# Attention output transposed on two column halves of TensorE, and moved by DMA into the first GEMM's input

## The chip, the cores and the metric

One core of one Trainium2 chip runs the whole program. The metric is the device time of one execution in microseconds (us); the kernel before took 1053.1 us, the median of 3 runs (1052.9 to 1053.57).

## The reference

What is computed, cut to what matters. The mixer is a linear recurrence for each of 4 batches and 8 heads over 768 tokens, with a complex decay for each of the 48 key dimensions; then come two MLPs.

```
B, H, S, D = 4, 8, 768, 48
for t in range(S):                        # state S is complex, D x D for each batch and head
    new_re = ar * S_re - ai * S_im
    new_im = ar * S_im + ai * S_re
    S_re, S_im = new_re + k[t] (x) v[t], new_im
    y[t] = q[t] @ S_re
x = y.transpose(0, 2, 1, 3).reshape(3072, 384)
h = x @ w_in                              # 384 -> 2048
x = (h * clip(h + 3, 0, 6) / 6) @ w_out   # 2048 -> 384
out = (((x @ w1) * (x @ w2)) @ w3) @ w_out2
```

## The kernel before, in words

**Numbers.** Each large GEMM works on operands split into a high part (fp32r, rounded) and a low part (the remainder), in three products: high by high, high by low, low by high. Such a matmul is one record of the trace. Attention's own matmuls are plain fp32; one of these is two weight loads and two matmul records.

**Tiling.** Tokens come in 24 chunks of 128 (`NC`), three chunks make a unit of 384 tokens (`UNIT`), and there are 8 units (`NU`). A batch has 6 chunks, so that chunks 0, 6, 12 and 18 (`c == 0`) have no state from before them.

**The outer loop.** Every engine's program is written out by hand over `units` (from -2 to 7) and 16 slots `sl` in each. In slot `sl` of unit `u`, TensorE does one step of the first GEMM (`gemm1`, 9 matmuls of 384 columns into `hb`) and, two steps behind, one step of the second (`gemm2`, 9 matmuls into `acc`). Between them, in `u`'s slots, stand the pieces of attention of unit `u + 1`. For its chunk j (0, 1, 2) they are, by the table `STAGE`: decay sums `D` in slot 4j, transposes of Q and K (`TQ`, `TK`) in 4j+2 and 4j+3, scores `Sc` in 4j+4, output `Y` and state update `U` in 4j+5, and `turn_x` in 4j+6. So units -2 and -1 are a start without GEMM steps, and 21 of the 24 chunks (3 to 23) lie among the GEMM steps of units 0 to 6. The last part, after unit 7, is the second MLP; it has no attention in it.

**What a chunk's output does before.** `Y(g, i)` does four heads: for each head, `bQ[:, h*48:(h+1)*48]` is the sum of QbT as weights (96 rows, 128 columns) with the state `Z` moving (48 columns), if c > 0, and of the masked scores `AT` as weights (128 by 128) with `v_sb` moving (48 columns). `Y(g, 0)` stands behind `gemm1`, `Y(g, 1)` behind `gemm2`, and `U(g)` (8 matmuls with 96 weight columns and 48 moving ones into `bR`) behind that. The result has tokens on its partitions. ScalarE copies it to `xs` (`y_copied`), `turn_x` turns it with three 128x128 transposes into bank `bP`, ScalarE writes the high part `xH` and VectorE the low part `xL`, which the next unit's `gemm1` reads.

**Around it.** Banks: `bQ` and `bR` serve Q's and K's transposes, scores, output and state update in turn; `bP` serves decay sums, angle sums and `turn_x`. `TQ` of the next chunk is one slot behind `YU` and waits for `y_copied` and `state_out` (VectorE's last operation on `Z`, in `z_out`). VectorE does in a `YU` slot, in this order: the product `g_sb`, `rot` of the next chunk (`Qb`, then `Kb`, which waits for `U`), `z_out`, and a stage `pre` of the decays of the unit after next. All DMAs are on the one queue of SyncE, in the order of its program.

## Time and profile before

| what | value |
|---|---|
| median of 3 runs | 1053.1 us (1052.9 to 1053.57) |
| span of the profiled execution (first to last instruction) | 1051.8 us |
| so outside the span, against the median | 1.3 us |
| PE (TensorE matmul) busy | 1006.4 us, 96% of the span |
| PEld (weight loads, beside the matmuls) | 931.9 us, 89% |
| DVE (VectorE) | 528.6 us, 50% |
| ACT (ScalarE) | 428.5 us, 41% |
| POOL (GpSimd) | 366.7 us, 35% |

PE's busy time counts each matmul until its modelled end, and matmuls overlap; the distance from one record's start to the next one's is what a matmul costs in a full stream. A row of the timeline that merges several records gives the start of the first.

### The profile page before, as it was taken

To read this page: it belongs to the slowest core of one execution; us is meant where nothing else is said; L and a number is where in the kernel's file an instruction comes from. 1 tells how busy PE (TensorE), PEld (TensorE's weight loads), DVE (VectorE), ACT (ScalarE), POOL (GpSimd) and SP (SyncE) were. 2 spreads that over 40 slices of the span, in tenths; PEclk is the share of its full clock that TensorE was granted. 3 is DMA by queue.
4 is the path that set the end of the run, shared out by engine and by line. 5 is a ranking of instruction groups with operands and counts; after the bars stand their busy time and mean duration, and the time that the engine had idled before them with its cause. 6 is when DMAs were issued, how large, how long until landed. Compare 5 with 4: busy or idle time off the path is not lost.

```text
span 1051.8 us, 15149 instructions
## 1 busy us (share of the span) xinstructions
PE 1006.4 (96%) x5985; PEld 931.9 (89%) x5985; DVE 528.6 (50%) x669; ACT 428.5 (41%) x698; POOL 366.7 (35%) x294
## 2 busy tenths in 40 slices
PE   6887799999999999999999999999999999999996
PEld 3566699999999999999999999999888888888886
DVE  4678568668668758667857754334212121212111
ACT  4373454455454464454454452254312121212221
POOL 0261353453452452463363442135212221222111
PEclk9997699999999999999999999999999999999999
DMA  9252210110110021021020010060101010101000
GB/s 354 74 179 68 82 39 23 54 61 24 53 54 30 11 83 44 9 83 35 20 84 25 29 39 23 9 232 1 53 1 61 1 60 1 60 1 61 1 31 32
DMA packets 35176, 57.42 MB, mean 55 GB/s; under 512 B 2592, under 2 KB 29472, under 8 KB 35104
## 3 DMA queue, kind: packets, MB, share of 16 engines
q1 hardware_dynamic: 35104, 56.42, 16.1%
q8 instruction: 50, 0.82, 0.3%
q14 instruction: 22, 0.18, 0.1%
HBM read 45.40 MB, written 11.01 MB: 54 GB/s over the span
## 4 chain that ended last, share of the span: by engine, by line
PE 84%; issue 5%; DVE 4%; ACT 3%; POOL 2%; DMA 1%; SPq 0%; ACTq 0%; POOLq 0%; DVEq 0%
PE acc L712 16%; PE hb L692 14%; PE hb L913 10%; PE acc L935 7%; PE bQ L913 5%; PE bR L913 5%; PE bQ L792 4%; PE bQ L791 3%; PE bR L799 3%; PE bP L935 2%; PE bR L776 2%; PE acc L860 2%; PE bQ L776 2%; POOL gL L1312 2%; DVE W L1172 1%
## 5 line engine op out<-in xcount | busy, mean ns | idle before, releaser
L1312 POOL TENSOR_TENSOR gL<-g_sb,gH 128x384 fp32r<-128x384 f32 x128 | 159.6, 1247 | 272.1 <-ACT gH L1013 272.1
L1360 POOL TENSOR_TENSOR pL<-p_sb,pH 128x512 fp32r<-128x512 f32 x48 | 67.0, 1396 | 231.9 <-ACT pH L1099 231.9
L712 PE MATMUL acc<-gH,woutH 128*128 128x384 f32 x384 | 131.5, 342 | 3.8 <-ACT gH L1013 2.3
L1231 DVE SCALAR_TENSOR_TENSOR g_sb<-t_sb,hb 128x384 f32<-128x384 f32 x128 | 70.3, 549 | 127.4 <-ACT t_sb L1031 69.5
L712 PE MATMUL acc<-gH,woutL 128*128 128x384 f32 x384 | 128.8, 335 | 0.0
L712 PE MATMUL acc<-gL,woutH 128*128 128x384 f32 x384 | 128.6, 335 | 0.0
L1031 ACT ACTIVATE t_sb<-hb,cst 128x384 f32<-128x384 f32 x128 | 74.6, 583 | 86.6 <-PE hb L692 85.5
L1013 ACT CAST gH<-g_sb 128x384 fp32r<-128x384 f32 x128 | 65.5, 512 | 88.5 <-DVE g_sb L1231 88.5
L692 PE MATMUL hb<-xH,winH 128*128 128x384 f32 x384 | 95.4, 356 | 0.0
L692 PE MATMUL hb<-xL,winH 128*128 128x384 f32 x384 | 88.5, 338 | 0.0
L692 PE MATMUL hb<-xH,winL 128*128 128x384 f32 x384 | 87.7, 336 | 0.0
L712 PEld LDWEIGHTS acc<-gH,woutH 128*128 128x128 f32 x384 | 72.2, 188 | 7.9 <-ACT gH L1013 4.0
L1289 DVE TENSOR_TENSOR p_sb<-a_sb,bQ 128x512 f32<-128x512 f32 x24 | 16.5, 688 | 111.7 <-PE bQ L913 95.9
L712 PEld LDWEIGHTS acc<-gL,woutH 128*128 128x128 f32 x384 | 72.2, 188 | 0.0
L712 PEld LDWEIGHTS acc<-gH,woutL 128*128 128x128 f32 x384 | 72.1, 188 | 0.0
L792 PE MATMUL bQ<-v_sb,AT 128*128 128x48 f32 x384 | 71.7, 280 | 0.0
L1091 ACT COPY a_sb<-hb 128x512 f32<-128x512 f32 x48 | 28.2, 588 | 104.2 <-PE hb L913 104.2
L692 PEld LDWEIGHTS hb<-xL,winH 128*128 128x128 f32 x384 | 69.9, 190 | 0.0
L692 PEld LDWEIGHTS hb<-xH,winL 128*128 128x128 f32 x384 | 69.1, 189 | 0.0
L1289 DVE TENSOR_TENSOR p_sb<-a_sb,bR 128x512 f32<-128x512 f32 x24 | 16.5, 687 | 104.7 <-PE bR L913 99.7
L692 PEld LDWEIGHTS hb<-xH,winH 128*128 128x128 f32 x384 | 65.3, 191 | 0.4
L1099 ACT CAST pH<-p_sb 128x512 fp32r<-128x512 f32 x48 | 29.8, 621 | 85.4 <-DVE p_sb L1289 85.4
(166 smaller groups left out, 2214.0 us busy)
## 6 DMA issues: line engine op xcount, KB each, us to landing
AR<-in_a_re_dram SPq DMA_DIRECT2D x8, 576.0 KB, 4.1
AI<-in_a_im_dram SPq DMA_DIRECT2D x8, 576.0 KB, 5.2
q_sb<-in_q_dram SPq DMA_DIRECT2D x24, 192.0 KB, 2.5
k_sb<-in_k_dram SPq DMA_DIRECT2D x24, 192.0 KB, 3.0
v_sb<-in_v_dram SPq DMA_DIRECT2D x24, 192.0 KB, 2.4
x_dram<-x_sb SPq DMA_DIRECT2D x24, 192.0 KB, 2.7
out_dram<-o_sb SPq DMA_DIRECT2D x6, 768.0 KB, 4.3
w3t_sb<-in_moe_w_dram SPq DMA_DIRECT2D x8, 512.0 KB, 8.5
```

Of the source, the lines that this page charges most:

```text
L692: mm = pe.matmul(o, w[:, kk * DF1 + ft * P:kk * DF1 + (ft + 1) * P], xv(x, u)[:, kk, :], start=(i == 0), stop=(i == 8))
L712: mm = pe.matmul(acc[m][:, 0:UNIT], w[:, ft * DM + m * P:ft * DM + (m + 1) * P], gg[:, (n % 3) * UNIT:(n % 3 + 1) * UNIT], start=(ft == 0 ...
L776: mm = pe.matmul(bk[:, hh * P:(hh + 1) * P], heads(KbT, h, P)[0:D2, :], heads(QbT, h, P)[0:D2, :], start=True, stop=True)
L792: mm = pe.matmul(o, heads(AT, h, P), heads(v_sb[:, :], h, D), start=(c == 0), stop=True)
L913: mm = pe.matmul(bk[n % 2][:, :], w[:, kk * DF2 + ft * P:kk * DF2 + (ft + 1) * P], x[:, o:o + UNIT2], start=(i == 0), stop=(i == 8))
L935: mm = pe.matmul(acc2[tb][:, 0:DM], pp[:, o:o + P], w[:, ft * DM:(ft + 1) * DM], start=(ft == 0 and i == 0), stop=(ft == FT2 - 1 and i == 2))
L1013: act.copy(gH[:, (n % 3) * UNIT:(n % 3 + 1) * UNIT], g_sb[:, :]).then_inc(s["hswish_high"], 1)
L1031: act.activation(t_sb[:, :], hb[n % 2][:, 0:UNIT], ACT.Relu, bias=THREE_C).then_inc(s["relu_done"], 1)
L1231: dve.scalar_tensor_tensor(out=g_sb[:, :], in0=t_sb[:, :], scalar=6.0, in1=hb[n % 2][:, 0:UNIT], op0=ALU.min, op1=ALU.mult).then_inc(s["hs ...
L1289: dve.tensor_tensor(p_sb[:, (n % 2) * UNIT2:(n % 2 + 1) * UNIT2], a_sb[:, (n % 2) * UNIT2:(n % 2 + 1) * UNIT2], bb[n % 2][:, :], ALU.mult) ...
L1312: pool.tensor_tensor(gL[:, (n % 3) * UNIT:(n % 3 + 1) * UNIT], g_sb[:, :], gH[:, (n % 3) * UNIT:(n % 3 + 1) * UNIT].bitcast(F32), ALU.subt ...
L1360: pool.tensor_tensor(pL[:, (n % 3) * UNIT2:(n % 3 + 1) * UNIT2], p_sb[:, (n % 2) * UNIT2:(n % 2 + 1) * UNIT2], pH[:, (n % 3) * UNIT2:(n % ...
```

## The change

The output of a chunk is computed transposed. For each pair of heads, the state `Z` (96 rows) and `v_sb` (128 rows) are now the weights, 64 columns of each head (48 and 16 more, which belong to the next head or to a cleared pad), and QbT and AT are the moving operand, 128 columns. The even head's result goes to partitions 0 to 63 of `bQ`, the odd head's to 64 to 127. All heads of a chunk stand in one block behind `gemm2`. ScalarE rounds the bank to a high part and VectorE takes the low part, both into `yHL`; `turn_x`, `xs` and their waits are gone, and so are `xH` and `xL` as separate copies from `bP`. Six DMAs a chunk, from SBUF to SBUF, bring the 48 rows of each head to their place in `xHL`; the rows of `w_in` are laid out in the matching order outside the kernel (`w_in_x`).

```diff
-        xH = at("xH", 2 * KT * UNIT, F32R)
-        xL = at("xL", 2 * KT * UNIT, F32R)
+        xHL = at("xHL", 4 * KT * UNIT, F32R)
...
-        xs = at("xs", DM)
+        yHL = at("yHL", H * P, F32R)
...
+            def store_x(g):
+
+                u, j = divmod(g, CPU)
+                sp.wait_ge(s["y_low"], g + 1)
+                y = yHL[:, :].bitcast(F32).rearrange("p (b n) -> p b n", n=P)
+                x = xv(u).bitcast(F32)[:, :, j * P:(j + 1) * P]
+                done = s[f"x_dma{u % 2}"]
+                sp.dma_start(x[0:D, 0:6, :], y[0:D, 0:6, :]).then_inc(done, 16)
+                sp.dma_start(x[D:D2, 0:6, :], y[YM:YM + D, 0:6, :]).then_inc(done, 16)
+                sp.dma_start(x[D2:P, 0:2, :], y[0:P - D2, 6:8, :]).then_inc(done, 16)
+                sp.dma_start(x[D2:P, 2:4, :], y[YM:YM + P - D2, 6:8, :]).then_inc(done, 16)
+                sp.dma_start(x[D2:D2 + 16, 4:6, :], y[P - D2:D, 6:8, :]).then_inc(done, 16)
+                sp.dma_start(x[D2 + 16:P, 4:6, :], y[YM + P - D2:YM + D, 6:8, :]).then_inc(done, 16)
...
                 if ft == 0:
-                    pe.wait_ge(s["xT_high"], CPU * (u + 1))
-                    pe.wait_ge(s["xT_low"], CPU * (u + 1))
+                    pe.wait_ge(s[f"x_dma{u % 2}"], 16 * XD * CPU * (u // 2 + 1))
...
                 pe.wait_ge(s["q_turned"], g + 1)
                 if g > 0:
-                    pe.wait_ge(s["y_copied"], g)
+                    pe.wait_ge(s["y_high"], g)
+                    pe.wait_ge(s["y_low"], g)
                     pe.wait_ge(s["state_out"], g)
...
-                for h in range(4 * i, 4 * i + 4):
-                    o = bQ[:, h * D:(h + 1) * D]
+                for pair in (2 * i, 2 * i + 1):
+                    o = [bQ[YM * r:YM * (r + 1), pair * P:(pair + 1) * P] for r in range(2)]
                     if c > 0:
-                        pe.matmul(o, heads(QbT, h, P)[0:D2, :], heads(Z, h, D)[0:D2, :], start=True, stop=False)
-                    mm = pe.matmul(o, heads(AT, h, P), heads(v_sb[:, :], h, D), start=(c == 0), stop=True)
+                        for r in range(2):
+                            h = 2 * pair + r
+                            pe.matmul(o[r], Z[0:D2, h * D:h * D + YM], heads(QbT, h, P)[0:D2, :], start=True, stop=False)
+                    for r in range(2):
+                        h = 2 * pair + r
+                        mm = pe.matmul(o[r], v_sb[:, h * D:h * D + YM], heads(AT, h, P), start=(c == 0), stop=True)
...
-            def turn_x(g):
...
+                    if n is not None and n >= 2:
+                        gemm2(n - 2)
                     if (g := chunk(u, sl, "YU")) is not None:
                         Y(g, 0)
-                    if n is not None and n >= 2:
-                        gemm2(n - 2)
-                    if g is not None:
                         Y(g, 1)
                         U(g)
...
-                        act.copy(xs[:, :], bQ[:, 0:DM]).then_inc(s["y_copied"], 1)
...
+                            act.wait_ge(s["y_low"], g)
+                            act.wait_ge(s[f"x_dma{(g - 1) // CPU % 2}"], x_landed(g - 1))
+                        act.copy(yv(0), bQ[:, :].rearrange("p (i n) -> p i n", n=P)).then_inc(s["y_high"], 1)
...
                         z_out(g)
-                    if (g := chunk(u, sl, "X")) is not None:
...
+                        dve.wait_ge(s["y_high"], g + 1)
+                        dve.tensor_tensor(yv(1), bQ[:, :].rearrange("p (i n) -> p i n", n=P), yv(0).bitcast(F32),
+                                          ALU.subtract).then_inc(s["y_low"], 1)
```

TensorE's order at a chunk with state (slot 5 of a unit), before: the last matmuls of `gemm1` (L692), then the first half of `Y` (L791 with the state, L792 with the scores; four heads), then `gemm2` (L712).

```order
L692 MATMUL hb<-xH,winL 128x384 x3
L791 MATMUL bQ<-Z,QbT 128x48 [waits s_state_in,s_v_dma,s_scores_masked]
L792 MATMUL bQ<-v_sb,AT 128x48
L791 MATMUL bQ<-Z,QbT 128x48
L792 MATMUL bQ<-v_sb,AT 128x48
L791 MATMUL bQ<-Z,QbT 128x48
L792 MATMUL bQ<-v_sb,AT 128x48
L791 MATMUL bQ<-Z,QbT 128x48
L792 MATMUL bQ<-v_sb,AT 128x48
L712 MATMUL acc<-gH,woutH 128x384 [waits s_hswish_low,s_hswish_high]
L712 MATMUL acc<-gL,woutH 128x384
```

The same place after the change: `gemm2` (now L737) stands ahead, and behind its last matmul comes the output (L820 with the state, L823 with the scores), two heads in turn.

```order
L737 MATMUL acc<-gH,woutH 128x384
L737 MATMUL acc<-gL,woutH 128x384
L737 MATMUL acc<-gH,woutL 128x384
L820 MATMUL bQ<-QbT,Z 64x128 [waits s_state_in,s_v_dma,s_scores_masked]
L820 MATMUL bQ<-QbT,Z 64x128
L823 MATMUL bQ<-AT,v_sb 64x128 x2
L820 MATMUL bQ<-QbT,Z 64x128 x2
L823 MATMUL bQ<-AT,v_sb 64x128 x2
```

So the first half of `Y` moved behind `gemm2`, and each of the 16 matmuls now writes 64 partitions by 128 columns where it wrote 128 by 48. VectorE's order in the same slot and the next one, after the change; L1256 is the new subtraction.

```order
L1191 TENSOR_TENSOR Kb<-cs,GK 128x768 [waits s_kv_summed,s_k_decayed]
L1213 TENSOR_TENSOR Z<-bR,Z 96x384 [waits s_kv_summed]
L1215 TENSOR_TENSOR Z<-Z,Et 96x384 [waits s_state_added]
L1256 TENSOR_TENSOR yHL<-bQ,yHL 128x4x128 [waits s_y_high]
L1124 TENSOR_TENSOR W_65<-W_65,W_66 128x1152 [waits s_ln_mag_capped,s_exp_ln_mag]
L1230 SCALAR_TENSOR_TENSOR g_sb<-t_sb,hb 128x384 [waits s_hswish_low,s_relu_done]
L1203 TENSOR_TENSOR Z<-Z,Et 96x384 [waits s_state_out,s_half_decays_T]
L1240 COPY QbT<-bR 96x512 [waits s_qT_psum]
```

Before, the subtraction of the low part (`xL`, 384 columns) stood behind `QbT` in the next slot; it now stands ahead of `pre`'s W in the chunk's own slot. SyncE's order at the end of a unit (slots 13 to 15), after the change; the six DMAs are new, the others stood there before.

```order
L602 DMA v_sb<-in_v_dram 128x384 [waits s_kv_summed]
L639 DMA xHL<-yHL 48x6x128 [waits s_y_low]
L640 DMA xHL<-yHL 48x6x128
L641 DMA xHL<-yHL 32x2x128
L642 DMA xHL<-yHL 32x2x128
L643 DMA xHL<-yHL 16x2x128
L644 DMA xHL<-yHL 16x2x128
L589 DMA AR<-in_a_re_dram 128x3x384 [waits s_turns_low,s_angles_summed]
L589 DMA AI<-in_a_im_dram 128x3x384
```

The six stand behind the load of the next chunk's V and ahead of the loads of a unit's decays.

## Rows read from the trace of the kernel before

**Rows 1.** The page, section 1: busy us (share of the span) xinstructions, by engine.

```profile
PE 1006.4 (96%) x5985; PEld 931.9 (89%) x5985; DVE 528.6 (50%) x669; ACT 428.5 (41%) x698; POOL 366.7 (35%) x294
```

**Rows 2.** Windows: stretch, length, busy by engine (xcount), PEclk, DMA share, GB/s.

```profile
0.00:98.00 98.00, 75.53 (x338) 51.54 (x338) 67.01 (x69) 50.59 (x62) 27.80 (x18) 0.94 0.50 173
98.00:127.00 29.00, 22.43 (x82) 19.47 (x83) 17.46 (x21) 9.35 (x14) 7.47 (x5) 0.56 0.33 102
455.40:537.30 81.90, 81.16 (x559) 79.75 (x559) 58.66 (x76) 41.07 (x72) 36.31 (x32) 1.00 0.14 44
```

**Rows 3.** PE's waits over the whole span: us in total, times, longest.

```profile
PE acc L712 <- ACT gH L1013: 2.3, 6, 0.4
PE bP L847 <- DVE xL L1259: 1.4, 1, 1.4
```

**Rows 4.** Timeline of PE in a chunk's slot: start, us, line, out<-in, xcount.

```profile
468.88 0.35 PE L791 MATMUL bQ<-Z,QbT 96*128 96x48 f32 x2
...
470.62 0.42 PE L712 MATMUL acc<-gH,woutH 128*128 128x384 f32 x1
...
470.88 0.34 PE L712 MATMUL acc<-gL,woutH 128*128 128x384 f32 x1
...
472.29 0.32 PE L791 MATMUL bQ<-Z,QbT 96*128 96x48 f32 x2
...
474.01 1.52 PE L799 MATMUL bR<-v_sb,Kb 128*96 128x48 f32 x16
...
475.36 0.78 PE L692 MATMUL hb<-xH,winH 128*128 128x384 f32 x3
```

**Rows 5.** Timeline of PE at `turn_x`, alone in its slot.

```profile
442.55 0.49 PE L818 MATMUL bP<-cst,xs 128*128 128x128 f32 x3
442.80 0.78 PE L692 MATMUL hb<-xH,winH 128*128 128x384 f32 x3
```

**Rows 6.** Timeline of PE at `TQ`: four transposes with 96 weight columns each.

```profile
457.13 0.60 PE L759 MATMUL bQ<-cst,Qb 128*96 128x128 f32 x4
457.57 0.60 PE L759 MATMUL bR<-cst,Qb 128*96 128x128 f32 x4
```

**Rows 7.** Timeline of PE at `halves_sums`: six matmuls with 32 weight columns, between others.

```profile
575.76 1.52 PE L799 MATMUL bR<-v_sb,Kb 128*96 128x48 f32 x16
577.11 0.35 PE L726 MATMUL bP<-logrH,cstR 128*32 128x384 f32 x1
...
578.17 0.68 PE L692 MATMUL hb<-xH,winH 128*128 128x384 f32 x3
```

**Rows 8.** Timeline of DVE and PE between a chunk's `U` and the next `TQ`.

```profile
475.64 0.96 DVE L1192 TENSOR_TENSOR Kb<-cs,GK 128x768 f32<-128x768 f32 x1 [2.02 <-PE bR L799]
...
477.10 0.79 DVE L1216 TENSOR_TENSOR Z<-Z,Et 96x384 f32<-96x384 f32 x1
...
478.59 0.60 PE L759 MATMUL bQ<-cst,Qb 128*96 128x128 f32 x4
```

**Rows 9.** Timeline from a unit's last `U` to the next unit's first `gemm1`.

```profile
520.51 0.42 PE L844 MATMUL bP<-TH,cstR 128*128 128x384 f32 x1
...
521.31 0.56 DVE L1216 TENSOR_TENSOR Z<-Z,Et 96x384 f32<-96x384 f32 x1
...
528.62 0.70 PE L692 MATMUL hb<-xH,winH 128*128 128x384 f32 x3
```

**Rows 10.** The DMA queue's packets, MB, share; one issue; one load's time to landing.

```profile
q1 hardware_dynamic: 35104, 56.42, 16.1%
...
476.41 0.43 SPq L587 DMA_DIRECT2D k_sb<-in_k_dram  x1
...
v_sb<-in_v_dram SPq DMA_DIRECT2D x24, 192.0 KB, 2.4
```

**Rows 11.** Timeline of PE at chunk 2 of the start, output and state update.

```profile
101.15 0.49 PE L791 MATMUL bQ<-Z,QbT 96*128 96x48 f32 x2
...
107.85 2.76 PE L799 MATMUL bR<-v_sb,Kb 128*96 128x48 f32 x16
```

More of the change, by code:

```diff
@@ L141, in mixer_mlp_kernel @@
         MID = cstR[:, 2 * P:3 * P]
-        HALF = [cstR[:, 3 * P + 32 * j:3 * P + 32 * (j + 1)] for j in range(CPU)]
+        HALF = [cstR[:, 3 * P + 2 * (CPU - 1 - j):3 * P + 2 * (CPU - 1 - j) + 32] for j in range(CPU)]
         w3t_sb = at("w3t_sb", FT2 * DF2, F32, wout_at)
@@ L258, in heads, with xv, x_landed, yv @@
             return t[:, h * w:(h + 1) * w]
-        def xv(t, u):
-            n = KT * UNIT
-            return t[:, (u % 2) * n:(u % 2 + 1) * n].rearrange("p (k n) -> p k n", k=KT)
+        def xv(u):
+            n = 2 * KT * UNIT
+            return xHL[:, (u % 2) * n:(u % 2 + 1) * n].rearrange("p (b n) -> p b n", n=UNIT)
+        def x_landed(g):
+            u, j = divmod(g, CPU)
+            return 16 * XD * (CPU * (u // 2) + j + 1)
+        def yv(part):
+            return yHL[:, :].rearrange("p (i c n) -> p i c n", c=2, n=P)[:, :, part, :]
         units = range(-2, NU)
@@ L642, in _ @@
                         load_v(g + 1)
+                    if (g := chunk(u, sl, "X")) is not None:
+                        store_x(g)
                     if sl == 15 and u + 3 < NU:
@@ L649, in _ @@
                     if u == NU - 2 and sl == 15:
-                        sp.wait_ge(s["xT_low"], NC)
-                        sp.wait_ge(s["xT_high"], NC)
+                        for i in range(2):
+                            sp.wait_ge(s[f"x_dma{i}"], 16 * XD * CPU * NU // 2)
                         sp.wait_ge(s["kv_summed"], NC)
@@ L689, in gemm1 @@
                 i = 0
-                for w, x in ((winH, xH), (winH, xL), (winL, xH)):
+                for w, part in ((winH, 0), (winH, 1), (winL, 0)):
                     for kk in range(KT):
-                        mm = pe.matmul(o, w[:, kk * DF1 + ft * P:kk * DF1 + (ft + 1) * P], xv(x, u)[:, kk, :],
+                        mm = pe.matmul(o, w[:, kk * DF1 + ft * P:kk * DF1 + (ft + 1) * P], xv(u)[:, 2 * kk + part, :],
                                        start=(i == 0), stop=(i == 8))
@@ L800, in U @@
                 mm.then_inc(s["kv_summed"], 1)
-            def turn_x(g):
-                a, j = divmod(g, CPU)
-                pe.wait_ge(s["y_copied"], g + 1)
-                if j == 1 and a + 1 < NU:
-                    pe.wait_ge(s["half_decays"], a + 2)
-                elif j < 2:
-                    pe.wait_ge(s["decays"], g + 2)
-                elif a == 0:
-                    pe.wait_ge(s["sin_turns"], CPU + 1)
-                elif a + 1 < NU:
-                    pe.wait_ge(s["sin_turns"], CPU * (a + 1) + 2)
-                else:
-                    pe.wait_ge(s["xT_low"], g)
-                for kk in range(KT):
-                    mm = pe.transpose(bP[:, kk * P:(kk + 1) * P], xs[:, kk * P:(kk + 1) * P], IDENT)
-                mm.then_inc(s["xT_psum"], 1)
             def angle_sums(p, j):
@@ L880, in _ @@
                     a, p = u + 1, u + 2
-                    for stage, do in (("D", decay_sums), ("TQ", TQ), ("TK", TK), ("S", Sc), ("X", turn_x)):
+                    for stage, do in (("D", decay_sums), ("TQ", TQ), ("TK", TK), ("S", Sc)):
                         g = chunk(u, sl, stage)
@@ L1305, in _ @@
             EARLY_LOW = (0, 12, 13)
+            for t in (v_sb, Z):
+                pool.memset(t[:, DM:DM + YM - D], 0.0).then_inc(s["pads_cleared"], 1)
             def low_g(n):
@@ L1371, in constants, with x_rows @@
     m = ((mid < src) & (src <= dst)).astype(np.float32) - ((dst < src) & (src <= mid)).astype(np.float32)
-    half = np.zeros((P, CPU, 32), np.float32)
-    for j in range(CPU):
-        half[:, j, 2 * j], half[:, j, 2 * j + 1] = i <= mid, i > mid
+    half = np.zeros((P, 32 + 2 * (CPU - 1)), np.float32)
+    half[:, 2 * (CPU - 1)], half[:, 2 * CPU - 1] = i <= mid, i > mid
     return np.concatenate([np.eye(P, dtype=np.float32), np.full((P, 1), 1.0, np.float32), np.full((P, 1), 3.0, np.float32),
-                           tri, np.ones((P, P), np.float32), m, half.reshape(P, CPU * 32)], 1)
+                           tri, np.ones((P, P), np.float32), m, half], 1)
+def x_rows():
+    rows = []
+    for kk, (h, e) in enumerate(((H - 2, 0), (H - 1, 0), (None, P - D2))):
+        rows += range(2 * kk * D, (2 * kk + 2) * D)
+        rows += (range(h * D, h * D + P - D2) if h is not None else
+                 [*range((H - 2) * D + e, (H - 1) * D), *range((H - 1) * D + e, H * D)])
+    return np.array(rows)
 def kernel(**inputs):
```

65 lines of the change are left out of this document (25 added, 40 removed).

## The prediction

> **What bounds the kernel now.** I read the page first, for who is busy: PE 96% of the span, the next engine (DVE) 50% [rows 1]. A mean over stages can mislead, so next the windows: over one whole unit (81.9 us, from one unit's slot 1 to the next one's) PE is busy for 81.16, DVE for 58.66, and the granted clock is 1.00, the 2.4 GHz level [rows 2]. PE's own waits come third: among the GEMM steps they are small, 2.3 us in six times for the largest [rows 3]. So in units 0 to 6 time is what TensorE's stream costs, and the timeline tells what a piece of it costs by the distance between starts, since records overlap.
>
> **The prices in the stream.** In a chunk with state, the output's first half takes 468.88 to 470.62, 1.74 us, and the second 472.29 to 474.01, 1.72 us: 3.46 us for 16 matmuls, that is 32 records of 108 ns [rows 4]. The state update has 16 records in 474.01 to 475.36, 1.35 us or 84 ns each [rows 4]. Both move only 48 columns; they differ in weight columns, 128 against 96. So weights set the pace, at 24 ns for 32 columns, and 64 columns would be 60 ns by the same line. A four-transpose group with 96 weight columns, which by weights would take 84 ns each, takes 0.44 us, 110 ns each [rows 6]: there the 128 moving columns set it. A transpose is one pass as one record of an fp32 matmul is, so I take 110 ns as the price of 128 moving columns.
>
> **The change, part by part.** Per matmul record it swaps 128 weight columns and 48 moving ones for 64 and 128.
>
> 1. *Output.* If the two halves of the array work at the same time, two records share 110 ns of moving, 55 each, and their weights take 60 each: weights set it, 32 x 60 = 1.92 us in place of 3.46. If not, a record is 110 ns and the output 3.52 us. No row of before has two column halves at work, so both ends stay for the range. The order written, even head, odd head, even, odd, lets a half's second record run beside the other's first, and weight loads already run beside matmuls in this trace (PEld 931.9 us beside PE 1006.4 [rows 1]). I take the first end, nearer to what these loads do: 1.54 us less a chunk, 0.77 where c = 0. Among GEMM steps there are 18 chunks with state and three without: 18 x 1.54 + 3 x 0.77 = 30.0 us.
>
> 2. *One block.* Each return from plain fp32 to a GEMM step costs 0.26 us to the second start (470.62 to 470.88) [rows 4] where 0.18 is the pace of these matmuls (six in 1.06 us [rows 7]): 0.08 us. One return a chunk goes: 21 x 0.08 = 1.7 us.
>
> 3. *turn_x.* 442.55 to 442.80, 0.25 us [rows 5], and 0.08 more where it stands alone, which is one of three: 0.28 on the mean, 21 x 0.28 = 5.9 us.
>
> 4. *Turning the array into halves and back*, 42 times. Nothing in before shows it for certain. The nearest row is the sum with 32 weight columns: it starts 1.35 us behind the state update's start, as long as that update takes anyway, and six of them with the return take 1.06 us, 0.18 each [rows 7]. That is zero, if those 32 columns run as a part of the array. The other end is a stream that has to run empty: a record's length over its pace, 0.34 less 0.18, up to the whole 0.34 [rows 4]. I take 0.16 x 42 = 6.7 us lost, between 0 and 14.
>
> The Trainium skill ("TensorEngine Tiling (Array Packing)", Key Properties) says that a change of tiling mode drains TensorE. By it the term is not zero; what a drain costs it doesn't say. The same skill ("TensorE: Matmul & The Clock Gate", Part 3, Measured speedup vs the span model) gives 2.38 times for three column tiles, 0.79 of ideal; for two at that rate, an estimate, a record would cost 69 ns, the output 2.21 us, and the whole 5.7 us less gain than mine. No run here shows it yet.
>
> 5. *New waits on bQ.* The next TQ now waits for the low part, behind ScalarE's rounding and VectorE's queue. At j = 0, counted from the end of U at 475.36 [rows 4]: Kb from 475.64, Z's last product ends at 477.89, and the subtraction over 512 columns adds about 0.75 (0.56 for 384 [rows 9], by columns): 478.64, where TQ starts at 478.59 [rows 8]. All of this hangs from U's end and moves with it, so TQ is some 0.2 us late with its semaphore, 7 x 0.2 = 1.4 us. At j = 1 halves_sums stands between, 1.06 us [rows 7], and covers it; at j = 2 the next TQ is five slots on. Behind the subtraction on VectorE are pre and the next g_sb, 0.75 later; the old subtraction behind QbT is gone, so the queue is only 0.2 longer a chunk, some 59 of 77.5 us. On ScalarE two operations become one. Without this cover each 0.1 us costs 0.7.
>
> 6. *The DMAs.* 8 blocks of 96 rows are 768 packets of 512 bytes a chunk. SyncE issues one in 0.43 us and a load of 192 KB lands in 2.4 [rows 10]. Chunks j = 0 and 1 have slots to spare. The last has not: from U's end (520.51) the low part is there at 521.87 + 0.75, so +2.1; six issues of 0.43 end at +4.7; the last lands 2.4 from its start, +6.7. The next unit's first gemm1 stood at +8.1 [rows 9], less turn_x 0.34: +7.8. Other bound: 35104 packets in 16.1% of 16 engines' span are 77 ns each [rows 10], 48 an engine are 3.7 us, all added to the first landing: 2.1 + 2.4 + 3.7 = +8.2. So between 1.1 us early and 0.4 late; at the last boundary, where no angle sums stand between (8 matmuls of 0.18), 1.4 less. I take 1.6 us in all, 0 to 5. Queued behind them on SyncE are the loads of decays, a unit ahead of their use, and V's load three slots on: nothing urgent.
>
> 7. *The start.* Chunks 0 to 2 lie before the GEMMs. Chunk 2's output takes 101.15 to 107.85, 6.70 us [rows 11], as the clock there is 0.56, near the 1.2 GHz level [rows 2]. At twice 60 ns a record it would be 3.84, 2.9 less; chunk 1 gives 1.5, chunk 0 0.8, the transposes 1.4 and the wait of an angle sum for xL 1.4 [rows 3]: 8.0 if all of it is on the path. But PE is busy only 75.53 of the first 98 us [rows 2], and weight splitting runs beside. I take half, 4.0, between 0 and 8.
>
> Sum: 30.0 + 1.7 + 5.9 - 6.7 - 1.4 - 1.6 + 4.0 = 31.9 us off the profiled span of 1051.8, so 1019.9; with the 1.3 us outside it, 1021 us against the median of 1053.1.
>
> **The rivals.** 0.2% of this time, 2.1 us, is about what a measurement can tell from no change.
>
> - *Halves overlap in part*, a record at 85 ns, midway: output 2.72 us, 0.74 less a chunk: 19.5 x 0.74 = 14.4 in place of 30.0, and a us less at the start: 1038 us. Two moving operands at a time is what no row shows.
> - *No overlap*, 110 ns: the output loses 19.5 x 0.06 = 1.2, parts 2 and 3 gain 7.6, parts 4 to 6 cost 9.7, the start gives 2: 1054 us, no change. For it: every record in the trace works alone on the array, and starts are in order.
> - *Slower: weights of a half aren't loaded ahead.* Then a record is 60 + 110 = 170 ns, the output 5.44 us, 19.5 x 1.98 = 38.6 lost, in place of 30.0 gained, and nothing at the start: 1094 us. It decides from 108 ns a record: there the output costs what it did, and the other terms cancel (7.6 - 9.7 + 2). Against it: PEld and PE are both busy 80 of 82 us in a unit [rows 2], so loads do run ahead, if with the whole array.
> - *The DMAs are late at each unit's end*, by 3 us rather than 0.2, if packets of this kind are much slower than 77 ns: 8 x 3 = 24 us, 1043 us. The packets of before speak against it [rows 10].
>
> The Trainium skill ("TensorE: Matmul & The Clock Gate", Part 3, The mechanism) has a rule for the slower one: weight loads overlap matmuls only when the row groups differ. Here both halves use all rows. The trace of before contradicts it for the whole array, since all its matmuls use the same rows [rows 2]; for halves no row shows it.
>
> **How the numbers follow.** Full overlap 0.60 (its own range 1011 to 1031, from parts 4 to 7's bounds); part overlap 0.15; none 0.11; weights in series 0.07; late DMAs 0.07. The likeliest is 1021. The range 1011 to 1048 takes in the first two and the late DMAs, and leaves out the other two. Faster: 0.60 + 0.15 + 0.06 of the late DMAs = 0.81; same, most of no overlap: 0.07; slower 0.12.
>
> **What would show it.** The new output's 32 records between gemm2's last start and U's first: near 1.9 us for my case, 3.5 for none, 5.4 for series. Even and odd head's records should lie on each other. The starts around the block, less pace, give part 4. TQ at slot 6 with a wait for yHL gives part 5, the first gemm1 of a unit with a wait for a DMA part 6. A unit should take about 77.5 us for 81.9. I am wrong if records stand 110 ns or more apart, or if gemm1 waits over 1 us at every unit.

## The result and the profile after

The changed kernel takes 1009.59 us, the median of 4 runs (1009.13 to 1010.04), against 1053.0 for the kernel before in the same session (1052.54 to 1053.57): ratio 0.9589, 95% interval 0.9578 to 0.96. That is 43 us less; the prediction said 1021, range 1011 to 1048. The mechanism was the one forecast, its size was not: the profiled span went from 1051.8 to 1007.3, 44.5 less, where 31.9 was worked out. The profiled execution of the changed kernel is its fastest, 1009.13, with 1.8 us outside the span, and in all other runs it is 1.7 to 2.0; by that measure the one of the kernel before is its slowest, 1053.57, and the 1.3 that the prediction took outside its span is 0.5 too small. So 1.1 us of the 44.5 is not in the medians.

The page of the changed kernel, busy times and the DMA queue (packets, MB, share of 16 engines), beside [rows 1, 10]:

```profile
PE 960.0 (95%) x5913; PEld 877.4 (87%) x5913; DVE 528.4 (52%) x669; ACT 422.3 (42%) x674; POOL 364.9 (36%) x296
...
q1 hardware_dynamic: 55840, 65.84, 20.5%
...
xHL<-yHL SPq DMA_DIRECT2D x48, 144.0 KB, 2.6
```

PE is still the bound, and 46 us of its busy time are gone. The largest of the new transfers land in 2.6 us (median).

Windows of the changed kernel: two whole units, then the three stretches of [rows 2] (the second stretch of [rows 2] had a granted clock of 0.56):

```profile
349.20:501.60 152.40, 150.89 (x1088) 145.72 (x1086) 114.98 (x150) 80.69 (x135) 71.66 (x63) 1.00 0.21 63
0.00:98.00 98.00, 73.77 (x338) 48.48 (x340) 67.38 (x72) 49.79 (x60) 28.30 (x20) 0.96 0.53 181
98.00:127.00 29.00, 21.27 (x123) 19.35 (x124) 23.69 (x25) 14.17 (x22) 17.94 (x12) 0.78 0.43 130
127.00:662.00 535.00, 529.55 (x3813) 511.72 (x3812) 371.07 (x488) 270.04 (x453) 232.03 (x206) 1.00 0.22 67
```

Two units take 152.4 us in place of 162.6, so the mean unit takes 76.2 in place of 81.3 (the 81.9 of [rows 2] is the longer unit of a pair). The granted clock is 1.00, the 2.4 GHz level, in both kernels among the GEMM steps from 127 us on; between 98 and 127 us it is 0.78 after the change.

The new block in the timeline of PE, in a chunk with state. The last `gemm2` matmul stands at 440.62, then come the output (L820 from the state, L823 from the scores), `U` (L830), and the return to `gemm1` (L717); 447.21 and 447.59 are the last `gemm2` matmul before the next `TQ`, and that `TQ`:

```profile
440.62 0.34 PE L737 MATMUL acc<-gH,woutL 128*128 128x384 f32 x1
440.88 0.44 PE L820 MATMUL bQ<-QbT,Z 96*64 96x128 f32 x4
441.15 0.39 PE L823 MATMUL bQ<-AT,v_sb 128*64 128x128 f32 x4
...
442.48 0.39 PE L823 MATMUL bQ<-AT,v_sb 128*64 128x128 f32 x4
442.79 1.56 PE L830 MATMUL bR<-v_sb,Kb 128*96 128x48 f32 x16
444.18 1.29 PE L717 MATMUL hb<-xHL,winH 128*128 128x384 f32 x6
...
447.21 0.34 PE L737 MATMUL acc<-gH,woutL 128*128 128x384 f32 x1
447.59 0.61 PE L784 MATMUL bQ<-cst,Qb 128*96 128x128 f32 x4
```

How to read it: the output's 32 records begin at 440.88 and `U` follows at 442.79, 1.91 us in place of 3.46 [rows 4]. Groups of four records start 0.22 us apart (441.15 to 442.48 is six groups in 1.33), 55 ns a record, half of the 110 ns that 128 moving columns cost in a transpose [rows 6]. A change of mode, from the whole array to halves or back, shows as the excess over the pace: 440.62 to 440.88 is 0.26 for 0.17, so 0.09 going in, and the last group takes 0.31 for 0.22, 0.09 coming out. `TQ` starts 0.38 behind the last matmul, 0.2 over the pace.

PE's waits after the change (us in total, times, longest):

```profile
PE hb L717 <- DMA xHL<-yHL: 3.9, 2, 3.3
...
PE bP L851 <- issue: 1.9, 4, 0.9
```

The new DMAs are waited for twice: 3.3 us ahead of the very first `gemm1`, and 0.6 ahead of the last unit. At the ordinary unit's end nothing is waited for: in the one from 482 us on, the state update ends at 485.78, the last of the six DMAs is issued at 491.03 and lands in some 1.9 us, and `gemm1` of the next unit starts at 493.52.

**Where the 44.5 us came from.** VectorE's evacuation of `acc` marks the end of each unit: in the kernel before at 211.5 (unit 0) and 694.1 (unit 6), after at 196.7 and 650.5. The first `gemm1` starts at 118.39 before and 110.19 after. So 8.2 us come ahead of the first `gemm1`, 6.6 more in unit 0, 28.8 in the six units after it, and 0.9 behind them, in a stretch that the change doesn't touch and that takes 356.5 to 357.7 us in all the profiles of this study. The prediction, split in the same way: 4.0, 4.0 (a seventh of its 27.9 among GEMM steps), 23.9 and 0.

Units come in pairs of different length; "two units" below is the time between the ends of units 1 and 3, which was 162.6 in the kernel before (292.2 to 454.8) and is 152.4 in the changed one (272.7 to 425.1).

### The profile page after: what moved, and what is told of

It is laid out like the page before. It is cut to its first block, busy times and chain, and to the rows that moved or that the text cites. A ratio compares the mean times of both kernels' runs of the same rounds, so it can differ in the third digit from the quotient of the medians.

```text
span 1007.3 us, 15116 instructions
## 1 busy us (share of the span) xinstructions
PE 960.0 (95%) x5913; PEld 877.4 (87%) x5913; DVE 528.4 (52%) x669; ACT 422.3 (42%) x674; POOL 364.9 (36%) x296
## 2 busy tenths in 40 slices
DMA packets 55913, 66.84 MB, mean 66 GB/s; under 512 B 4896, under 2 KB 50208, under 8 KB 55840
## 3 DMA queue, kind: packets, MB, share of 16 engines
q1 hardware_dynamic: 55840, 65.84, 20.5%
## 4 chain that ended last, share of the span: by engine, by line
PE 80%; issue 7%; DVE 5%; ACT 3%; POOL 3%; DMA 1%; SPq 1%; ACTq 0%; POOLq 0%; DVEq 0%
PE acc L737 15%; PE hb L717 14%; PE hb L916 10%; PE acc L938 8%; PE bR L916 5%; PE bQ L916 5%; PE bR L830 3%; POOL gL L1310 3%; PE bP L938 2%; PE bR L801 2%; PE acc L864 2%; PE bQ L801 2%; PE bQ L823 2%; PE bQ L820 2%; PE bQ L784 1%
## 5 line engine op out<-in xcount | busy, mean ns | idle before, releaser
L1310 POOL TENSOR_TENSOR gL<-g_sb,gH 128x384 fp32r<-128x384 f32 x128 | 155.4, 1214 | 253.5 <-ACT gH L1016 209.5
L717 PE MATMUL hb<-xHL,winH 128*128 128x384 f32 x768 | 162.8, 347 | 3.9 <-DMA xHL<-yHL 3.9
L717 PEld LDWEIGHTS hb<-xHL,winH 128*128 128x128 f32 x768 | 133.6, 191 | 5.0 <-DMA xHL<-yHL 4.6
L737 PE MATMUL acc<-gH,woutH 128*128 128x384 f32 x384 | 129.1, 336 | 4.1 <-ACT gH L1016 2.6
L737 PE MATMUL acc<-gH,woutL 128*128 128x384 f32 x384 | 128.6, 335 | 0.0
L737 PE MATMUL acc<-gL,woutH 128*128 128x384 f32 x384 | 128.3, 334 | 0.0
L717 PE MATMUL hb<-xHL,winL 128*128 128x384 f32 x384 | 87.7, 336 | 0.0
L737 PEld LDWEIGHTS acc<-gH,woutH 128*128 128x128 f32 x384 | 72.1, 188 | 6.9 <-ACT gH L1016 4.3
L737 PEld LDWEIGHTS acc<-gL,woutH 128*128 128x128 f32 x384 | 72.1, 188 | 0.0
L737 PEld LDWEIGHTS acc<-gH,woutL 128*128 128x128 f32 x384 | 72.1, 188 | 0.0
L717 PEld LDWEIGHTS hb<-xHL,winL 128*128 128x128 f32 x384 | 69.3, 189 | 0.0
L1323 POOL TENSOR_TENSOR GQ<-GQ,q_sb 128x384 f32<-128x384 f32 x24 | 24.3, 1011 | 82.2 <-ACT GK L1008 78.5
L938 PE MATMUL acc<-woH,pL 128*128 128x384 f32 x144 | 48.7, 338 | 0.0
L938 PE MATMUL acc<-woH,pH 128*128 128x384 f32 x144 | 48.6, 338 | 0.0
```

Of the source, the lines that this page charges most:

```text
L717: mm = pe.matmul(o, w[:, kk * DF1 + ft * P:kk * DF1 + (ft + 1) * P], xv(u)[:, 2 * kk + part, :], start=(i == 0), stop=(i == 8))
L737: mm = pe.matmul(acc[m][:, 0:UNIT], w[:, ft * DM + m * P:ft * DM + (m + 1) * P], gg[:, (n % 3) * UNIT:(n % 3 + 1) * UNIT], start=(ft == 0 ...
L938: mm = pe.matmul(acc2[tb][:, 0:DM], pp[:, o:o + P], w[:, ft * DM:(ft + 1) * DM], start=(ft == 0 and i == 0), stop=(ft == FT2 - 1 and i == 2))
L1310: pool.tensor_tensor(gL[:, (n % 3) * UNIT:(n % 3 + 1) * UNIT], g_sb[:, :], gH[:, (n % 3) * UNIT:(n % 3 + 1) * UNIT].bitcast(F32), ALU.subt ...
```

## The experiments

Each was timed in five rounds or more against the kernel before, whose median in these sessions was 1052.3 (experiments 1, 3, 4 and 9), 1052.7 (5, 7, 8 and 10) and 1053.2 (2, 6 and 11). An interval behind a ratio is the 95% interval. "Two units" and "unit 0" are read from the one profiled execution of each kernel. The start varies by itself: the kernel before and experiment 5 have the same program ahead of the first GEMM step and the same order of the two engines in experiment 8, and chunk 2's output begins at 101.15 us in one and at 99.95 in the other. So a difference of a us or so at the start tells nothing.

**1. The two halves: even heads, then odd heads, within each four.**

```diff
-                for pair in (2 * i, 2 * i + 1):
-                    ... (both heads of a pair in turn)
+                for r in range(2):
+                    for pair in (2 * i, 2 * i + 1):
+                        ... (one head at a time, two of a half in a row)
```

> The changed kernel with another order inside the output block: four even-head matmuls on the lower column half, then four odd-head ones on the upper, instead of even and odd alternating. Same matmuls, same number. If the gain of the output comes from both halves working at once, this order undoes most of it: records 110 ns apart except at the changes of half, some 3.3 us a block for 1.8, so 1.5 us for each of 18 chunks, 0.7 for each of 3, and the start: about 1040 us. If the halves need not overlap and the smaller weights alone made it cheaper, it stays at 1010.

1021.45 us (1020.25 to 1022.67), ratio 0.9702 (0.9689 to 0.9715). Neither end. Timeline of PE in this kernel, the whole output block (L820 from the state, L821 from the scores):

```profile
448.73 0.43 PE L820 MATMUL bQ<-QbT,Z 96*64 96x128 f32 x2
449.00 0.38 PE L821 MATMUL bQ<-AT,v_sb 128*64 128x128 f32 x2
449.22 0.44 PE L820 MATMUL bQ<-QbT,Z 96*64 96x128 f32 x4
449.44 0.44 PE L821 MATMUL bQ<-AT,v_sb 128*64 128x128 f32 x4
...
450.93 0.38 PE L821 MATMUL bQ<-AT,v_sb 128*64 128x128 f32 x2
451.24 1.56 PE L828 MATMUL bR<-v_sb,Kb 128*96 128x48 f32 x16
```

In the program the first eight records are all one half's. In the trace only the first four stand alone (448.73 and 449.00, two records in 0.22, so 110 ns each); from 449.22 groups of four start 0.22 to 0.28 apart, nearly as many as two halves at work give. The odd half's first matmul began four records ahead of its turn. The block takes 2.51 us, 0.60 more than 1.91, and two units take 155.5 (277.5 to 433.0), 3.1 more. Of the six chunks in two units one is the first of its batch (`c == 0`) and has half the output, so 5.5 x 0.60 = 3.3 is what the rows give.

**2. All even heads of the chunk, then all odd ones** (the wait for the masked scores of all eight heads now stands ahead of both).

```diff
-                for pair in (2 * i, 2 * i + 1):
+                for pair in range(4):
+                    r = i
```

> The changed kernel with all even heads (one column half) of a chunk's output first, 16 records, and then all odd heads, 16 records. With four even and four odd records in turn the halves still ran beside each other, one some four records behind. Theory A, TensorE looks ahead over a few instructions only, so that halves 16 records apart can't lie on each other except at the seam: most of the 32 records then cost 110 ns, the output some 3.3 to 3.5 us in place of 1.9, 19.5 x 1.5 = 29 us and 2 or 3 at the start, 1040 us; and as PE then stays 4.6 us in plain fp32 matmuls a chunk, the clock may fall in mid-kernel as it did with one long block of the old output, which would make it longer still. Rival B, it looks as far ahead as its queue goes: as with halves in turn, 1021 us or less.

1036.84 us (1035.92 to 1041.12), ratio 0.9852 (0.9834 to 0.9871). Theory A holds: the output goes back to 3.28 us. Timeline of PE in this kernel:

```profile
424.96 0.43 PE L820 MATMUL bQ<-QbT,Z 96*64 96x128 f32 x2
425.23 0.38 PE L821 MATMUL bQ<-AT,v_sb 128*64 128x128 f32 x2
...
426.33 0.44 PE L820 MATMUL bQ<-QbT,Z 96*64 96x128 f32 x4
426.55 0.44 PE L821 MATMUL bQ<-AT,v_sb 128*64 128x128 f32 x4
426.82 0.38 PE L820 MATMUL bQ<-QbT,Z 96*64 96x128 f32 x2
...
428.24 1.56 PE L828 MATMUL bR<-v_sb,Kb 128*96 128x48 f32 x16
```

Two records in 0.22 nearly everywhere, 110 ns each; only at the seam (426.33 to 426.82) do eight records share 0.49 us, the last four of one half and the first four of the other. TensorE ran some four records ahead of the order, no more, in both kernels. Two units take 159.7 (285.7 to 445.4), 7.3 more than in the changed kernel, for 5.5 x 1.37 = 7.5 by the rows, and the window of that stretch shows the clock at 1.00. This is nearly the whole worth of the overlap: 19.5 x 1.37 = 27 us, with all else of the change in place.

**3. 48 weight columns rather than 64** (`v_sb[:, h * D:(h + 1) * D]` and the same of `Z`).

> The changed kernel with 48 weight columns for each head instead of 64, so without the 16 that belong to the next head; the rows they filled in the bank are not used by anything. In the changed kernel a record takes 55 ns. If the 128 moving columns of two records at a time set that (110 halved), nothing changes: 1009.6, same. If the 64 weight columns set it, as the prediction had it, a record goes to about 45 ns at most and the time falls by 0.3 us a chunk, 6 us: 1004.

1011.31 us (1008.93 to 1013.07), ratio 0.9602 (0.9588 to 0.9617). The interval overlaps that of the changed kernel, and two units take 152.4 (276.2 to 428.6), as in the changed kernel. So the 128 moving columns set the 55 ns, and a line from weight columns had nothing to say here. The profiled run was later at its start alone (end of unit 0 at 200.3 for 196.7), of which experiment 8 tells more.

**4. The output in two blocks again, around `gemm2`.**

```diff
-                    if n is not None and n >= 2:
-                        gemm2(n - 2)
                     if (g := chunk(u, sl, "YU")) is not None:
                         Y(g, 0)
+                    if n is not None and n >= 2:
+                        gemm2(n - 2)
+                    if g is not None:
                         Y(g, 1)
```

> The changed kernel with the first half of the output put back ahead of the second GEMM's step, as before the change; the second half stays behind it. It adds two changes between whole array and halves for each of 21 chunks and nothing else. The trace of the changed kernel shows about 0.09 us extra at the way in and 0.14 to 0.2 at the way out. If that is the price: 21 x 0.25 = 5 us, 1015 us. If a change costs nothing: 1010. If it drains for a record's whole length each way: 21 x 0.7 = 15 us, 1024.

1019.03 us (1017.63 to 1019.64), ratio 0.9681 (0.9667 to 0.9694). Two units take 154.4 (276.3 to 430.7), 2.0 more, or 0.33 a chunk for a second pair of changes and one return, 7 us over 21 chunks. Predicted were 0.32 and 0.08; the expectation of 0.25 a chunk, 1015 us, was too low, and a drain of a whole record each way, 1024, too high. The profile's end of unit 0 is 2.5 us later (199.2), of which experiment 8 tells more.

**5. The one block alone: the kernel before, with its old output in one block behind `gemm2`** (the same edit, the other way round).

> The kernel before with one part of the change alone: all eight heads of a chunk's output behind the second GEMM's step. It takes away one return from plain fp32 to a GEMM step a chunk, 21 x 0.08 = 1.7 us: 1051.3. If the first half ahead of that step had hidden a wait for the second GEMM's operands, it loses as much or more: 1053 to 1056.

1070.12 us (1067.37 to 1074.24), ratio 1.0169 (1.0148 to 1.019). A miss of both: 17 us slower, not 2 faster. Windows of 2 us in this kernel (PE busy, the others, then the granted clock, DMA share, GB/s); the output stands at 309.28 to 312.78 and `U` at 312.78 to 315.05:

```profile
310.00:312.00 2.00, 2.00 (x21) 2.00 (x20) 1.04 (x3) 0.20 (x1) 0.96 (x1) 1.00 0.00 0
312.00:314.00 2.00, 2.00 (x19) 2.00 (x18) 0.49 (x1) 1.02 (x2) 0.00 (x0) 0.77 0.00 0
314.00:316.00 2.00, 2.00 (x11) 2.00 (x11) 0.63 (x1) 1.01 (x2) 0.91 (x1) 0.50 0.00 0
...
320.00:322.00 2.00, 2.00 (x17) 1.95 (x16) 0.60 (x2) 0.69 (x2) 0.00 (x0) 1.00 0.00 0
```

PE is busy 2.00 of 2.00 us throughout, and the clock falls to the 1.2 GHz level at 313.1, 0.3 us into the state update, and stays there until 319.9: for 6.8 us, 4.8 of them GEMM steps. What PE did before it fell: 3.8 us of plain fp32 matmuls that move 48 columns each, the output and the first records of `U` in one piece. In the kernel before, a `gemm2` stood between the halves of that piece. This happens in some chunks, not all: its units take 82.0, 88.1, 80.6, 86.4, 80.6 and 79.8 us, where those of the kernel before take 80.7, 81.9, 80.7, 81.9, 80.6 and 76.8.

**6. Each output matmul twice, in the changed kernel** (`for pair in (2 * i, 2 * i + 1) * 2`; the second time into the same place).

> The changed kernel with each output matmul of a chunk issued twice (the second time into the same place, from the start again; the output is the same). It adds 32 records at the pace of the new form and no change of mode. Theory A, what lets the clock fall in the one long block of the old form is matmuls that move few columns, not the length of the plain fp32 stretch: the new form moves 128 columns in two halves, the granted clock stays at the 2.4 GHz level in units 0 to 6, and the kernel takes 19.5 x 1.76 = 34 us more, and 2 to 5 at the start: 1046 us. Rival B, the length of the stretch away from the GEMM steps decides (now some 5 us a chunk, as in the one long block of before): the clock falls in some chunks and the time is 1055 us or more.

1049.58 us (1046.65 to 1051.12), ratio 0.9966 (0.9956 to 0.9977). Theory A holds. Two units take 162.1 (288.6 to 450.7), 9.7 more. By 1.76 us (32 x 55 ns) it should be 5.5 x 1.76 = 9.7. Windows of 100 us in this kernel:

```profile
200.00:300.00 100.00, 99.00 (x735) 95.84 (x734) 69.86 (x89) 49.80 (x86) 49.70 (x41) 1.00 0.22 70
...
400.00:500.00 100.00, 99.24 (x810) 95.59 (x809) 73.69 (x92) 48.17 (x79) 40.77 (x36) 1.00 0.20 58
```

Output and `U` together now take 5.1 us a chunk (3.7 and 1.4), longer than the 3.8 after which the clock fell in experiment 5, in plain fp32 as there, and the clock doesn't move. It doesn't in experiment 2 either (3.28 and 1.4), where the halves work one at a time. So the length of the stretch away from the GEMM steps doesn't explain the fall. What differs from experiment 5 is the form of the output, 128 moving and 64 weight columns a record in place of 48 and 128; no run changes one of the two alone. The 3.5 us beyond the expectation are at the start: in this profile the first `gemm1` stands 7.5 us later than in the changed kernel (117.66 for 110.19) and the end of unit 0 11.5, with the slow order of experiment 8.

**7. `turn_x` twice, in the kernel before** (its three transposes issued again into the same place).

> The kernel before with turn_x's three transposes issued twice, same operands, same bank. What it adds is what one turn_x costs in the stream. At 0.25 us from the trace: 21 x 0.25 = 5.3 us among the GEMM steps and up to 1.4 at the start: 1058 to 1060. If transposes hide beside something, 1053 to 1055, and the gain of the change has to come from elsewhere.

1060.4 us (1059.72 to 1061.3), ratio 1.0074 (1.006 to 1.0088). The six units behind unit 0 take 488.2 (213.1 to 701.3) for 482.6 (211.5 to 694.1): 5.6 us over 18 chunks, 0.31 each, for 0.28 predicted. The end of unit 0 is 1.6 later. The forecast of 1058 to 1060 is met, and the term confirmed.

**8. Which of two engines goes first at the start.** In the profile of the kernel before, GpSimd's split of a `w_out` piece (L336) began 0.4 us ahead of VectorE's low part of the turns. Timeline of both engines there:

```profile
94.53 4.47 DVE L1159 TENSOR_TENSOR TL<-W,TH 128x1152 fp32r<-128x1152 f32 x1
...
94.14 3.64 POOL L336 TENSOR_TENSOR woutL<-wstage,woutH 128x1536 fp32r<-128x1536 f32 x1 [15.55 <-ACT woutH L331]
```

The same two in the changed kernel:

```profile
94.84 1.36 DVE L1158 TENSOR_TENSOR TL<-W,TH 128x1152 fp32r<-128x1152 f32 x1
...
94.83 4.68 POOL L346 TENSOR_TENSOR woutL<-wstage,woutH 128x1536 fp32r<-128x1536 f32 x1 [13.55 <-ACT woutH L341]
```

The subtraction takes 4.47 us in the first and 1.36 in the second, where the GpSimd operation is longer instead. In the first, GpSimd's ends at 94.14 + 3.64 = 97.78 and the subtraction 1.2 us behind that, at 99.00, as if it had begun only then. The order in which VectorE waits is called the slow one here, the other the quick one. An angle sum on PE starts right behind it: 4.05 us idle ahead of 99.10 before, 0.95 ahead of 96.30 after. The Trainium skill ("SBUF — State Buffer", SBUF: two separate sides) says that VectorE with two SBUF inputs and GpSimd share a port pair that one of them holds for its whole instruction; both traces agree, with 3.1 us more for VectorE in the first and 1.0 for GpSimd in the second (4.68 for 3.64). Which of the two goes first the starts don't always tell: in the changed kernel they are 0.01 us apart (94.83, 94.84) and VectorE had the quick way; in experiment 1 they are 0.01 apart too (92.92, 92.93) and its subtraction took 4.63. The experiment makes GpSimd wait for that subtraction:

```diff
                         if SPLIT_W[i] == (u, sl) and i not in SPLIT_DVE:
+                            if i == 4:
+                                pool.wait_ge(s["turns_low"], 2)
                             split_L(pool, i)
```

> The kernel before, with GpSimd made to wait, before the low part of the fifth piece of the first MLP's weights (slot 11 of unit -1), until VectorE has written TL of unit 1. In the trace of before GpSimd's 3.6 us subtraction began 0.4 us ahead of VectorE's TL and TL took 4.47 us; in the changed kernel they began together and TL took 1.36. TensorE then stood idle 4.05 us in before and 0.95 after, and its clock was at the lower level from 97 to 120 us in before and only some 13 us in all around there after. If this chance order at the start is what gave the part of the gain that the prediction missed: 5 to 9 us less, 1044 to 1048. If not, 1051 to 1054.

1049.68 us (1049.08 to 1050.22), ratio 0.9969 (0.9957 to 0.9981): 3.05 us less. The subtraction takes 1.36 there, PE's idle time ahead of the angle sum is gone (it starts at 96.39), the end of unit 0 comes 2.7 earlier (208.8). So the order is worth some 3 us, not the 5 to 9 that I asked of it.

**9. The low part of the output ahead of `Kb` and `Z` on VectorE, in the changed kernel** (a `low_y(g)` between the two operand blocks of `rot`, in place of its place behind `z_out`).

> The changed kernel with VectorE's subtraction for the low part put ahead of Kb and of the state update in its queue, so that it runs while TensorE is still at U. It should take away TQ's 0.2 us wait at j = 0 (7 of them), let the DMAs into the first GEMM's input start some 2 us earlier, and take away most of the first GEMM step's 3.3 us wait at the start and 0.6 at the last unit. If those waits are on the path: 3 to 5 us less, 1005 to 1007. If the start is bound elsewhere (the splitting of weights): 1.5 to 2 us less, 1008.

1006.36 us (1004.39 to 1007.55), ratio 0.9556 (0.9543 to 0.9569), 3.2 less than the changed kernel. The unit before the last boundary takes 71.3 for 72.9. Nothing stands there between a chunk's `U` and the next `gemm1`, and two waits of the changed kernel are gone: twice 0.34 us that `TQ` was late for the low part (600.17, 620.43) and 0.8 at the boundary for the DMAs. The five units ahead of it give 0.4 us together, and the end of unit 0 is 0.4 earlier, with the slow order of experiment 8 in this profile (the subtraction took 4.63 us).

**10. Experiments 8 and 9 together, on the changed kernel.**

> The changed kernel with both: the low part first on VectorE, and GpSimd's weight piece behind TL. If the changed kernel already has the good order at the start, the second adds nothing to the first: the same as with the low part first alone, within 1 us. If the good order was luck that a shift can lose, this one keeps it where the other may lose 5 to 8 us.

1004.44 us (1004.41 to 1005.39), ratio 0.9544 (0.9531 to 0.9557): 1.9 less than experiment 9, whose interval it overlaps, the end of unit 0 at 193.5 for 196.3, and the lowest median of the study.

**11. The output twice in chunks 0 to 2 alone, which lie ahead of the GEMM steps** (`* (2 if g < CPU else 1)`).

> The changed kernel with the output matmuls issued twice in chunks 0 to 2 alone, which lie before the GEMM steps. Theory A, the start gains more than the output's own shorter work, since a shorter output lets the clock come back: with 1.8 us more work in each of chunks 1 and 2 the clock stays near 1.2 GHz for longer, as it did in the kernel before, and the time is 7 to 12 us longer, 1017 to 1021 us. Rival B, only the work itself counts: 0.9 + 1.8 + 1.8 at the high level, up to twice that at the low one, of which what lies behind weight splitting is hidden: 1011 to 1015 us.

1016.3 us (1015.28 to 1017.29), ratio 0.9647 (0.9634 to 0.966), 6.7 more than the changed kernel: between the two ranges. Timeline of PE in this kernel, chunk 2 (L820, L823), `U` (L830):

```profile
102.77 1.62 PE L851 MATMUL bP<-TS,cstR 128*128 128x384 f32 x2 [4.21 <-issue]
...
104.95 0.70 PE L820 MATMUL bQ<-QbT,Z 96*64 96x128 f32 x4
...
107.57 0.46 PE L820 MATMUL bQ<-QbT,Z 96*64 96x128 f32 x4
107.86 0.39 PE L823 MATMUL bQ<-AT,v_sb 128*64 128x128 f32 x4
...
109.93 1.56 PE L830 MATMUL bR<-v_sb,Kb 128*96 128x48 f32 x16
```

A group of four takes 0.43 us up to 107.57 and 0.22 from 107.86: the clock comes back within the output, some 2.8 us after its start. So theory A is wrong in its reason: more of this work doesn't hold the clock down. The 7.9 us by which the end of unit 0 is late (204.6 for 196.7) are the order of experiment 8, which fell the other way here (4.21 us idle), some 3, chunk 2's 1.85 more (4.98 for 3.13), and, as what is left, some 3 for chunks 0 and 1.

## Why the prediction was wrong, step by step

The start and the stream each gave some 6 us more than the sum had, both in the same direction; the mechanism, two halves at work at once, is borne out. In the order written, 55 ns a record leaves no room for the rivals' 85, 110 or 170. Of the start's 6 us about half is luck: the two profiled executions differ in which of two engines went first.

- **Part 1, the output.** The step that failed: "their weights take 60 each: weights set it". A record takes 55 ns, the moving time shared by two halves, and with 48 weight columns it takes the same (experiment 3). The prediction's other estimate, 69 ns, is further off. The line through 48-column matmuls said how fast weights could be loaded there, but not that they would bind here. The 32 records take 1.76 us in place of 1.92, 0.16 less a chunk with state, which makes some 3 us. That both halves do work at once, the assumption with the widest bounds, held: 27 us hang on it (experiment 2), near the 30.0 of the sum. They even do so out of program order, by four records (experiments 1 and 2), so "starts are in order" was no argument for the rival without overlap.
- **Part 4, changes of mode.** From where the stream was due (440.62 + 0.17) to `U` are 2.00 us; less the 32 records that is 0.24 for two changes (0.09 going in, 0.05 more in the first group, 0.09 coming out), where 0.32 was taken. A second pair with its return costs 0.33 (experiment 4), for 0.40. Right in kind, 1.7 us too dear in all (21 x 0.08).
- **Part 2, one block.** The 1.7 us for a return is inside experiment 4's 0.33 and wasn't measured alone. What the part left out is larger: one block of the *old* output would have cost 17 us by the clock (experiment 5). The change has both parts at once and doesn't meet it.
- **Part 3, `turn_x`.** 0.31 us a chunk for 0.28 (experiment 7), 0.6 us in all.
- **Part 5, `TQ`.** 0.2 us late at j = 0 in units 0, 2 and 4 (447.21 to 447.59 above), on time in units 1, 3 and 5, whose chunk is the first of its batch and has half the output, and 0.34 late twice in unit 6, at j = 1 too, where no `halves_sums` stands between. That is 1.3 us for 1.4: the total came out, the places didn't.
- **Part 6, the DMAs.** 1.6 us were taken, 0.2 a unit. The trace shows no such wait at the ordinary unit's end; at the last boundary there is one, 0.8 from where `gemm1` was due (643.91, behind a last `gemm2` matmul at 642.96). So 0.8 was too much, and the rival of late DMAs is refuted. The terms together are 3.1 + 1.7 + 0.6 + 0.1 + 0.8 = 6.3, about the 5.7 that the stream gave more.
- **Parts 1 to 6 together**: 28.8 us in six units, 1.60 a chunk, for 1.33; over seven units 33.6 for 27.9.
- **Part 7, the start: the larger miss.** 8.2 us ahead of the first `gemm1` and, with 4.8 of unit 0's 6.6 taken as its stream (three chunks of 1.60), 1.8 behind it: 10.0 for 4.0 in these two profiles. The step that failed: "At twice 60 ns a record it would be 3.84, 2.9 less", and then "I take half". It left the clock where it stood in the kernel before. Timeline of PE in the changed kernel, chunk 2, for the 101.15 and 107.85 of [rows 11]:

```profile
96.30 0.96 PE L851 MATMUL bP<-TS,cstR 128*128 128x384 f32 x2 [0.95 <-issue]
...
97.83 0.70 PE L820 MATMUL bQ<-QbT,Z 96*64 96x128 f32 x4
...
100.02 0.57 PE L823 MATMUL bQ<-AT,v_sb 128*64 128x128 f32 x4
100.42 0.39 PE L820 MATMUL bQ<-QbT,Z 96*64 96x128 f32 x4
...
100.96 1.56 PE L830 MATMUL bR<-v_sb,Kb 128*96 128x48 f32 x16
102.35 0.88 PE L851 MATMUL bP<-TS,cstR 128*128 128x384 f32 x2
...
110.19 2.29 PE L717 MATMUL hb<-xHL,winH 128*128 128x384 f32 x6 [3.32 <-DMA xHL<-yHL]
```

Windows of 2 us around it, the changed kernel:

```profile
98.00:100.00 2.00, 2.00 (x20) 2.00 (x22) 1.90 (x4) 0.00 (x0) 2.00 (x2) 0.50 0.00 0
100.00:102.00 2.00, 2.00 (x28) 1.83 (x25) 2.00 (x2) 0.90 (x2) 0.58 (x1) 0.90 0.48 88
102.00:104.00 2.00, 1.58 (x11) 0.99 (x9) 1.97 (x4) 1.90 (x3) 0.33 (x1) 1.00 0.91 319
```

and the kernel before:

```profile
102.00:104.00 2.00, 2.00 (x11) 2.00 (x11) 1.93 (x4) 0.00 (x0) 0.43 (x1) 0.50 0.01 3
...
108.00:110.00 2.00, 2.00 (x15) 2.00 (x14) 0.00 (x0) 1.88 (x3) 0.00 (x0) 0.50 0.53 199
```

Both are at the 1.2 GHz level when chunk 2's output begins, and PE is busy all the time through it in both. In the old form, which moves 48 columns a record, the clock stays there through 6.70 us of output and the state update, until 120. In the new one it comes back after 2.6 us, at 100.4. The other profiles say the same. In experiments 1 to 4, 6, 9 and 11 the new output also begins at the low level, and the clock comes back 1.8 to 2.8 us into it, in experiment 2 too, where the halves work one at a time; in experiments 5, 7 and 8 the old one stays at the low level to its end and through the state update. In the changed kernel the clock fell once more at 107.2, while PE waited for the DMAs, and was low until 114.0, for the first 3.8 us of GEMM steps. Output and `U` take 4.52 us (97.83 to 102.35) in place of 9.26 (101.15 to 110.41): 4.7 less where 2.9 was reckoned (3.57 by the output and 1.17 by `U`, which the sum had left as it was). Another 3.3 us lie ahead of the output's start, nearly all of it the order of experiment 8 (4.05 less 0.95 of idle time), which this change of the output was not meant to set, and which varies between kernels that have it: it fell the slow way, with the subtraction at 4.6 us, in the profiles of experiments 1 to 4, 6, 9 and 11, and the quick way, without an added wait, in that of the changed kernel alone. What the output of chunks 0 and 1 gave, 2.3 us of the sum, can't be told from a start that varies by 1 us; experiment 11 shows that work there is at least partly on the path. What `turn_x` and the wait for `xL` were to give back, 2.8 by the sum, the first `gemm1`'s wait for its DMAs took again, 3.32.

Profiles of one order can be set side by side. The slow way: the kernel before and experiment 3, which has the changed kernel's stream, with spans of 1051.8 and 1011.2 and the end of unit 0 at 211.5 and 200.3. The quick way: experiment 8 and the changed kernel, 1048.4 and 1007.3, 208.8 and 196.7. So with the order held the change gives 40.6 and 41.1 us, and 11.2 and 12.1 by the end of unit 0; less 4.8 of stream, the start gives 6.4 and 7.3 for the 4.0 of the sum, and some 3 us of the profiled 44.5 are the order's. Had it not changed, the result would stand near 1012, an estimate from these spans, inside the range by a hair; experiment 3 took 1011.31.

What stays open: how much the order gave in the timed runs. Experiments 8 and 10 give 3 and 1.9 us for a fixed order, but only a profiled run shows which way it went. Why the clock comes back in the one form and not in the other is not shown beyond what the two forms do.

## What to carry to other kernels

A small fp32 matmul cost here its moving columns (110 ns a record for 128) or its weight columns (108 ns for 128), whichever took longer; two column halves that take turns share the moving time, and it pays to write them in turn, since TensorE runs only some four fp32 records ahead of the order. Before costing work at a low clock, ask whether the new form of that work brings the clock back; and before gathering short matmuls into one block, ask whether it sends the clock down among the GEMM steps, which cost the old form 17 us here without PE standing idle for it. Where several engines share a start, compare profiles in which the same engine went first, because which of two gets ahead by less than a microsecond is worth 3.
